# A fused attention and mixture-of-experts kernel on one core: a token-key multiply moves from VectorE to GpSimd, and part of a filler becomes quarter-array matmuls

## The reference

```python
for t in range(S):
    kt, vt, rt = (k[:, :, t], v[:, :, t], r[:, :, t])
    cur = np.einsum('bhd,bhe->bhde', u[None] * kt, vt)
    y[:, :, t] = np.einsum('bhd,bhde->bhe', rt, state + cur)
    state = w[None, :, :, None] * state + np.einsum('bhd,bhe->bhde', kt, vt)
```

```python
gate = 1.0 / (1.0 + np.exp(-(x @ w_gate)))      # 384 -> 1536
x = (gate * (x @ w_val)) @ w_out                # 1536 -> 384
...
logits = xn @ en.T / tau                        # cosine with 8 expert embeddings
expert_idx = np.argmax(logits, axis=1)
h = np.maximum(x[mask] @ w1[e], 0.0)            # 384 -> 1024
out[mask] = gate_w[mask, None] * (h @ w2[e])    # 1024 -> 384
```

## Time and profile before

| what | us |
|---|---|
| median of three runs | 885.38 |
| lowest, highest | 884.51, 886.44 |
| the profiled execution | 885.38 |
| its span in the profile | 883.7 |
| PE busy | 844.0 |
| POOL busy | 392.5 |
| DVE busy | 454.4 |
| ACT busy | 303.3 |

### The profile page before, as it was taken

One profiled execution on the slowest core, in us unless ns is written; L12 is line 12 of the kernel. 1 busy time (PEld: TensorE's weight loads), 2 busy tenths in 40 slices (PEclk: granted clock), 3 DMA queues, 4 the chain that ended last, 5 costly groups with the idle time before them and its releaser, 6 DMA issues.

```text
span 883.7 us, 20524 instructions
## 1 busy us (share of the span) xinstructions
PE 844.0 (96%) x7508; PEld 795.6 (90%) x7509; DVE 454.4 (51%) x1075; ACT 303.3 (34%) x622; POOL 392.5 (44%) x428
## 2 busy tenths in 40 slices
PE   6899999999999999999999999998999999999995
PEld 5788998998999999999999999987999999999995
DVE  6855456456446546545545633376367366366100
ACT  1532232232233223223213223333454454454442
POOL 3643325316315415315415413326566566566544
PEclk9769999999999999999999999999999999999998
DMA  9532302302212212212212210036354354354110
GB/s 286 185 115 75 94 19 83 93 20 83 75 39 65 80 43 73 75 47 74 74 48 73 69 46 19 16 128 180 115 156 146 94 160 146 90 164 137 58 35 29
DMA packets 76021, 79.68 MB, mean 90 GB/s; under 512 B 5720, under 2 KB 73248, under 8 KB 75952
## 3 DMA queue, kind: packets, MB, share of 16 engines
q1 hardware_dynamic: 62800, 57.93, 21.8%
q10 hardware_dynamic: 9216, 9.55, 3.8%
q0 software_dynamic: 3936, 11.23, 3.4%
HBM read 67.47 MB, written 12.01 MB: 90 GB/s over the span
## 4 chain that ended last, share of the span: by engine, by line
PE 90%; DVE 3%; issue 3%; ACT 1%; DMA 1%; POOL 0%; ACTq 0%; SPq 0%; POOLq 0%; DVEq 0%
PE ps L1269 35%; PE ps L1286 16%; PE ps L1382 13%; PE ps L1367 13%; PE ps L1390 3%; PE ps L1218 2%; PE ps L1197 2%; PE ps L1226 1%; PE ps L1202 1%; PE ps L1347 1%; PE ps L1232 1%; PE ps L1308 1%; DVE weights L1076 1%; PE ps L1239 1%; PE ps L1331 0%
## 5 line engine op out<-in xcount | busy, mean ns | idle before, releaser
L1269 PE MATMUL ps<-x_groups,weights 128*128 128x384 f32 x1728 | 318.0, 340 | 0.0
L1269 PEld LDWEIGHTS ps<-x_groups,weights 128*128 128x128 f32 x1728 | 300.0, 189 | 1.9
L564 POOL TENSOR_TENSOR hT<-gate,hT 128x384 fp32r<-128x384 f32 x96 | 98.5, 1029 | 170.0 <-ACT hT L702 170.0
L1286 PE MATMUL ps<-weights,hT 128*128 128x392 f32 x864 | 160.6, 344 | 0.0
L1286 PEld LDWEIGHTS ps<-weights,hT 128*128 128x128 f32 x864 | 152.6, 188 | 0.4
L1382 PE MATMUL ps<-weights,hT 128*128 x672 | 124.2, 339 | 1.7 <-ACT h_f L804 1.7
L1367 PE MATMUL ps<-weights,x_groups 128*128 (+1 forms) x504 | 122.8, 397 | 1.2 <-issue 1.2
L1033 DVE TENSOR_TENSOR gate<-ps,gate 128x384 f32<-128x384 f32 x96 | 53.3, 555 | 128.4 <-PE ps L1269 122.0
L1382 PEld LDWEIGHTS ps<-weights,hT 128*128 128x128 f32 x672 | 116.0, 188 | 1.9 <-issue 1.9
L1367 PEld LDWEIGHTS ps<-weights,x_groups 128*128 128x128 f32 x504 | 92.6, 188 | 20.5 <-issue 1.6
L1019 DVE CAST weights<-staged 128x768 fp32r<-128x768 f32 x56 | 47.7, 852 | 92.2 <-PE ps L1367 56.0
(11 more groups left out here) (181 smaller groups left out, 1005.3 us busy)
## 6 DMA issues: line engine op xcount, KB each, us to landing
staged<-in_moe_w SPq DMA_DIRECT2D x60, 384.0 KB
r_in<-routed ACTq DMA_DIRECT2D x30, 192.5 KB
rk_raw<-in_rt SPq DMA_DIRECT2D x21, 256.0 KB, 3.7
rk_raw<-in_kt SPq DMA_DIRECT2D x21, 256.0 KB, 3.8
r_in<-in_r SPq DMA_DIRECT2D x21, 192.0 KB, 2.4
k_in<-in_k SPq DMA_DIRECT2D x21, 192.0 KB, 3.9
v_in<-in_v SPq DMA_DIRECT2D x21, 192.0 KB, 2.4
first_raw<-in_moe_w_out SPq DMA_DIRECT2D x6, 384.0 KB, 13.5
```

What stands on the lines that cost most here:

```text
L564: g.tensor_tensor(hT_lo[:, f, :], gate[:, f % 2, :], hT_hi[:, f, :].bitcast(F32), ALU.subtract).then_inc(hlo_ready, 1)
L1269: ins = te.matmul(ps[:, bank[f % 2], 0:GT], wt[:, c, fs], x[:, half, c, :], start=(c == 0 and m == 0), stop=(c == KC - 1 and m == 2))
L1286: ins = te.matmul(ps[:, BX2[i], 0:XW], h[:, f, ts], wt[:, f, :], start=(f == 0 and m == 0), stop=(f == FC - 1 and m == 2))
```

## The change

The k_tok multiply leaves DVE. `scale_tokens` is gone, in tile 0 and in all others. On POOL it stands in stage 0 between the two bonus multiplies L531 and L537, in every one of the 24 tiles; in tile 0 it comes behind the power for the embeddings' norm (L535) and waits for `pow_ready`. Since k_tok has one buffer, POOL's stage 0 now waits for PE's stage 1 of the tile before (`scores`). PE's wait for `consts` in tile 0 goes. Of the 36 fillers ahead of `turn_rows(0)`, 12 and 8 stay whole; between them stand 48 that use a 64x64 quarter of the array in turn, 32 of them with 48 columns and 16 with 128.

```diff
                     if not (isinstance(T, int) and T == 0):
                         pool.wait_ge(y_turned, T)
+                        pool.wait_ge(scores, T)
                     g.tensor_tensor(bonus[:, :, :], k_t[:, :, :], r_t[:, :, :], ALU.mult).then_inc(rk_step, 1)
                     if isinstance(T, int) and T == 0:
                         pool.wait_ge(small_in, 48)
                         pool.wait_ge(en_squares, 1)
                         g.tensor_tensor(tiny[0:E, 5:6], tiny[0:E, 1:2], one_half[0:E, :], ALU.pow).then_inc(en_norm, 1)
+                        pool.wait_ge(pow_ready, 1)
+                    g.tensor_tensor(k_tok[:, :, 0:D], k_t[:, :, :], pow_tok[:, :, :], ALU.mult).then_inc(k_tok_ready, 1)
...
-            def scale_tokens(T):
-                dve.wait_ge(*arrival(T))
-                ve.tensor_tensor(k_tok[:, :, 0:D], tile_inputs(T)[1][:, :, :], pow_tok[:, :, :],
-                                 ALU.mult).then_inc(k_tok_ready, 1)
-
...
                     ve.tensor_tensor(rT[:, :, :], rk_raw[:, c % 2, 0, :, :], pow_r[:, :, :], ALU.mult).then_inc(rk_scaled, 1)
-                    if not (isinstance(T, int) and T == 0):
-                        scale_tokens(T)
...
-            dve.wait_ge(pow_ready, 1)
-            scale_tokens(0)
...
-                    if start:
-                        pe.wait_ge(consts, 6)
-                    else:
+                    if not start:
                         pe.wait_ge(y_ready, T)
...
+            def keep_clock_quarters(n, wide):
+
+                for i in range(n):
+                    across, down = i % 2, (i // 2 + i) % 2
+                    te.matmul(ps[HALVES[across], BT + down, 2 * P:2 * P + wide], ident[HALVES[down], 0:HP],
+                              ident[HALVES[down], 0:wide], start=True, stop=True)
...
-            keep_clock(BT, 36)
+            keep_clock(BT, 12)
+            keep_clock_quarters(32, D)
+            keep_clock_quarters(16, P)
+            keep_clock(BT, 8)
             turn_rows(0)
             keep_clock(BT, 14)
```

## The result

The changed kernel takes 892.32 us (median of 4; 891.9 to 893.3) against 885.5 us before it on the same chip (4 runs), a ratio of 1.0079 (95% interval 1.0061 to 1.0096): 0.8% slower. The forecast was 889.6, with a range up to 893.0.

A forecast was written before the change was run, and what follows sets the result against it. PE's own work was taken to bound the kernel, so only gaps on PE count: 885.38 + 5.2 (startup) - 5.3 (steady) - 0.5 (tile 3) + 3.4 (heads) + 1.4 (filler) = 889.6 us, range 885.3 to 893.0.

The forecast's parts named there:

- Startup: Tiles 0 to 2: k_tok queues behind POOL's other work, PE at half clock, first hidden_step at 59.6; +5.2 us, bounds +2.0 and +6.0.
- a little sooner: Tile 1: POOL's L531 would end near 30.15 instead of 30.6, since DVE is ahead by 0.5 us.
- startup rival: Startup runs at full clock and faster than before, -1.0 us there, 883.4 us in all; chance 0.12.
- Steady tiles: Middle and last tiles of groups, 14 of them: PE's 0.38 us wait before stage 1 vanishes, -5.3 us.
- tile 3: First steady tile, no scatter ahead on POOL: PE waits for rT alone, -0.5 us of the 0.76 idle.
- Heads: Six first tiles of groups: k_tok stands behind the scatter and L531 on POOL, PE 0.57 us later each, +3.4 us.
- The filler: Between dense and expert stage: filler over early at 597.4, clock lost, following fillers at half clock; +1.4 us, bounds 0 and +3.4.
- upper bound of no overlap at all: In the filler: the 16 quarters of 128 columns take up to 3.7 us if none overlap; 1.0 was taken.
- the term of 1.4: Behind the filler: the 14 fillers after turn_rows and following matmuls run at half clock until it returns, +1.4 us.
- The rival that has the clock at half for longer: Clock stays at half behind the filler through the first expert matmuls, +3.4 instead of +1.4, 891.6 us; chance 0.13.
- The rival of 888.2: The clock outlives the filler's gap, so the 1.4 us goes, 888.2 us; chance 0.17.
- POOL keeps the port: In the 14 steady tiles kT or rT lets one more POOL job pass, +8.1 instead of -5.3, 903.0 us; chance 0.06.

The follow-up runs named there:

- e1: k_tok on POOL in all 24 tiles with the old filler of 36 whole matmuls, otherwise the kernel before: 886.74 us, ratio 1.0014.
- e8: The kernel before with k_tok on POOL in tiles 1 and 2 alone, old filler: 889.64 us, ratio 1.0057.
- e3: The kernel before with k_tok on POOL from tile 3 on, on DVE in tiles 0 to 2, old filler: 882.25 us, ratio 0.9955.
- e4: The kernel before with k_tok on POOL from tile 3 on except in the six group heads from tile 6, old filler: 879.58 us, ratio 0.9932.
- e9: The kernel before, its filler unchanged, with the 48 quarters put twice into the dense stage, behind step 8 of groups 2 and 4: 888.53 us, ratio 1.0047.
- e5: The kernel before with 20 whole fillers instead of 36 ahead of the first rows and no quarters: 885.73 us, ratio 1.0015.
- e12: The kernel before with its old filler, but four of POOL's pad scatters moved behind POOL's part of the first rows: 891.39 us, ratio 1.0084.
- e7: The kernel before with a filler of 12 whole matmuls, 16 quarters of 128 columns and 20 whole: 884.28 us, ratio 0.9998.
- e6: The kernel before with the new filler, its 48 quarters replaced by as many full-array matmuls of the same 48 and 128 columns: 893.8 us, ratio 1.0090.
- e2: The kernel before with the new filler alone, k_tok staying on DVE: 891.49 us, ratio 1.0079.

## Why the prediction was right or wrong

**The time.** 889.6 was forecast, 892.3 measured, in the forecast's direction and inside the range, 0.7 us from its end. (The two upper bounds named for that end, 6.0 for the startup and 3.4 for the filler, add up to 892.4 and not 893.0.) That it is inside is in part luck, for the terms behind it fell out differently: the filler's was five times too small, and the steady part was better than forecast. The parts measured alone add up to +8.2 (5.2 - 4.0 + 7.0), the whole is +7.0, with an interval from 5.4 to 8.5.

**Startup, +5.2 forecast: 5.2 and 5.0 measured.** The step (k_tok behind two splits and L532, PE at half clock behind the idle) is right. In e1, whose profiled execution lies near its median, the intermediate times are those of the forecast: PE's stage 1 of tile 1 at 31.69 (31.25 forecast), the first dense step at 59.54 (59.6). In the changed kernel's slower profiled execution they are later, 33.83 and 62.11. There the second split waited for ACT's part and began at 29.29 instead of 26.61; PE's granted clock was 0.50 from 17.6 to 27.6, where it was 1.00 from 22.5 on before, and the transposes of weights that ACT copies took 0.80 to 0.85 us for three instead of 0.49 to 0.55. That this is what made ACT late was not tried by itself. That POOL comes "a little sooner" was wrong there. In tile 0 the power starts 0.5 us earlier as said, but k_tok and the bonus multiply then hold DVE's small multiply (L936, 1.73 us for 8 numbers, 0.77 before), and the embeddings' transpose comes at 17.24 instead of 16.77. The startup rival (883.4) is refuted by e8: with nothing won elsewhere the startup costs 5.0 us.

**Steady tiles, -5.3, tile 3, -0.5.** The idle vanished in all fourteen and in tile 3; the tile period fell by 0.44 us, not 0.38, so 14 x 0.44 = 6.2. The term counted only the idle in front of stage 1; where the other 0.06 comes from I haven't traced. e3 (which has this and the heads) measured -4.0 where -2.4 was the sum, with an interval of -2.7 to -5.3.

**Heads, +3.4.** The idle grew from 0.81 to 1.35, 0.54 instead of 0.57 each: 6 x 0.54 = 3.2. In time, e4 against e3 gives 2.0 by the ratios and 2.7 by the medians, somewhat less; their two intervals overlap, so the size in time is rough. The mechanism is as written: L580, L532, k_tok, PE 0.1 us later.

**The filler, +1.4 forecast (bounds 0 to 3.4): 7.0 measured.** This is the step that failed. I priced the quarters by L1202, 32 of whose records run at full speed, and took the block for shorter than its predecessor, so that the danger was an idle PE behind it. Both prices hold by themselves (e9: 2.04 us; e5: +1.3). What I left out is that nothing in L1202 tells how 96 short records in a row fare beside POOL's run of indirect DMAs; the nearest row had a third of the length and no such neighbour. The block took longer, not shorter: 48 quarters were 10.5 us long (597.91 to 608.44) where the sum had 2.3. The rows' arrival, which I took for what ends the wait, had happened: POOL copied from them at 604.88, PE turned them at 611.69. My upper bound of no overlap at all (3.7 us for 16) bounded the array's work and nothing else that can hold PE. A small sign stood in the trace of before and I read past it. Timeline of the kernel before, PE behind the first rows:

```profile
603.22 1.97 PE L1308 MATMUL ps<-ident 128*128 128x128 f32 x16 [0.60 <-issue]
```

An idle with no releaser in the middle of fillers that wait for nothing, ending 0.5 us after POOL's copy: it looks like the same stall at a tenth of the size.

**The clock, and the two rivals about it.** I forecast full clock until about 597 and half from 601, behind an early filler. Half clock from 601 came true for another reason, inside the stall (stretch, us, busy by engine, granted clock, DMA share, GB/s):

```profile
594.40:595.40 1.00, 1.00 (x7) 1.00 (x6) 0.89 (x7) 0.38 (x2) 0.50 (x1) 0.50 0.00 0
...
605.50:608.30 2.80, 2.31 (x41) 1.86 (x40) 1.99 (x3) 0.00 (x0) 0.21 (x1) 0.50 0.61 160
```

The clock was at 0.50 from 594.4 to 597.7, at 1.00 to 601.1, at 0.50 to 611.4 and at 1.00 from there, so the 14 fillers behind the rows ran at full clock and the term of 1.4 is nothing in this kernel. The rival that has the clock at half for longer names 891.6, the nearest of all to the measured 892.3, and is wrong all the same: its 3.4 us behind the filler didn't occur. The rival of 888.2, in which the term of 1.4 is gone, is right about the term and misses the stall. The first of the two stretches at half begins 1 us behind an idle of 1.92 us ahead of L1244. In the kernel before, e1, e8 and e9 the clock stayed full behind that same idle (2.10 us in e8; 72 filler records in 8.28 us); in the changed kernel and all others it fell, and in e3, e4 and e12 that is with the old filler (72 in 9.91). With the old filler this is hidden, since PE waits for the rows anyway (1.96 us before); e7 lost the clock there too and costs nothing.

**POOL keeps the port (903.0)** is refuted: kT and rT took 2.23 us together in tile 4 (2.35 before), and the idle of the 14 tiles is gone. The Trainium skill's Perfetto Trace Analysis, "Optimizing Scalar/DVE Operations", warns that a move between these two engines might not help; here it helps where PE was waiting for the third job in DVE's row, by 6.0 us in e4.

## What to carry to other kernels

Move work to another engine only in those repetitions in which its new queue is free: the same edit gave -6.0 us in 15 tiles, and lost 5 us in two tiles of the startup and some 2 to 3 in six heads. An idle with no releaser inside work that waits for nothing is a warning: something that the profile doesn't name holds the engine there. Here a long row of very short matmuls made it ten times as long, and the same matmuls broken up with long ones had none. When a moved piece of work removes a stall in the trace but not in the time, time the move by itself: its control showed that it paid the gain back.

## What was not expected of the hardware

- 96 short matmul records in a row beside a run of eight indirect DMAs on POOL: 41 at full speed, then one to three about every 0.7 us until the run and POOL's copy behind it were over, 7 us, then the rest. The same records took 2.04 us in the dense stage and 2.06 us beside a run of four.
- A full-array fp32 matmul of 48 columns took 0.11 us a record at a granted clock of 1.00 and 0.21 at 0.50 (e6), as much as one of 128 columns (e2 has both levels too).
- The same idle of about 1.9 us ahead of the filler was followed by a fall of the granted clock to 0.50 in ten kernels and not in three (before, e1, e9), with nothing else changed on PE between before and e12.
- A DVE multiply of 8 numbers took 1.73 us while POOL's k_tok and bonus multiply ran, and 0.77 beside the bonus multiply alone.
